# Routing digits counted with the comparisons as the stationary operand, the token list made a digit sooner, output products respread, and other orders at the seam between two experts layers

## The reference

```python
# 1. block-local attention, B=4, H=8, S=768, D=64: chunks of 32 queries see 16 left, 8 right, and 8 memory keys
# 2. mixture of experts 1: x [3072, 512], E=8, F=1024, cap = 3072 // 8 = 384
logits = x @ w_gate
order = np.argsort(-logits.flatten())
for idx in order:                                  # greedy, best logit first
    tok, e = (int(idx) // E, int(idx) % E)
    if assigned[tok] >= 0 or counts[e] >= cap:
        continue
    assigned[tok] = e
    counts[e] += 1
for e in range(E):
    out[assigned == e] = np.maximum(x[assigned == e] @ w1[e], 0.0) @ w2[e]
# 3. mixture of experts 2: noisy top-2 gating on the output of layer 2, no cap
noisy = logits + np.log1p(np.exp(x @ w_noise)) * noise
# softmax over the two best; out[token] += weight * (relu(x @ w1[e]) @ w2[e]) for each of its two experts
```

## Time and profile before

| | |
|---|---|
| time, 3 runs | 1354.14 us median (1353.6 to 1357.26) |
| profiled execution | 1354.46 us, of it 1352.7 us in the span of the profile |
| granted TensorE clock, mean | 0.959 |
| busy | PE 1241.1 us (92%), DVE 928.7 (69%), ACT 572.6 (42%), POOL 293.1 (22%) |
| attention, then the gate of layer 2 | 0 to 203 us of the span |
| routing steps n=0 and n=1 | 203 to 238, 238 to 289 us |
| routing steps n=2 to 6 | 289 to 559 us |
| `step_seventh`, `step_eighth`, `last_step` | 559 to 679 us |
| early tiles 0 and 1 of layer 3 | 679 to 730 us |
| other tiles | 730 to 1347 us, of which PE is busy 597.25 of the last 601 us |

### The profile page before, as it was taken

The page is one execution under the profiler, slowest core; times in us unless marked ns, Lnnn a source line. Parts: engine busy times, 40 slices in busy tenths (PEclk is TensorE's granted clock), DMA queues, the critical chain, the costliest instruction groups (busy, mean ns, idle before and its releaser), DMA issues.

```text
span 1352.7 us, 27991 instructions
## 1 busy us (share of the span) xinstructions
PE 1241.1 (92%) x9694; PEld 1101.9 (81%) x9694; DVE 928.7 (69%) x1924; ACT 572.6 (42%) x1232; POOL 293.1 (22%) x338
## 2 busy tenths in 40 slices
PE   7999982289999998989998999999999999999997
PEld 6888871277787876878897999898999999998986
DVE  4777756788877878754787666666666666666662
ACT  4666650133333322424323445444545455444541
POOL 3000000201102022030104324242423233232421
PEclk9999995589999999999999999999999999999999
DMA  8888853432432342444314315124252513334210
GB/s 141 165 165 164 167 129 141 141 110 80 139 111 78 132 130 72 140 150 139 87 37 157 109 55 180 40 84 144 72 175 65 196 54 116 112 103 153 80 42 18
DMA packets 174299, 154.66 MB, mean 114 GB/s; under 512 B 105117, under 2 KB 137885, under 8 KB 174240
## 3 DMA queue, kind: packets, MB, share of 16 engines
q1 hardware_dynamic: 151552, 102.83, 27.9%
q0 software_dynamic: 16128, 44.56, 10.8%
q10 hardware_dynamic: 6560, 6.49, 1.4%
HBM read 206.13 MB, written 33.75 MB: 177 GB/s over the span
## 4 chain that ended last, share of the span: by engine, by line
issue 37%; PE 33%; DVE 12%; POOL 10%; DMA 5%; ACT 2%; POOLq 1%; DVEq 0%; ACTq 0%
PE bank L784 7%; PE bank L764 6%; POOL partial L419 3%; DMA out<-result,token_now 3%; PE bank L640 3%; POOL out L423 3%; PE bank L649 2%; PE bank L628 2%; POOL held L399 2%; PE bank L710 2%; PE bank L664 2%; DMA xg<-x_dram,token_of 2%; POOL x L403 2%; PE bank L657 1%; PE bank L728 1%
## 5 line engine op out<-in xcount | busy, mean ns | idle before, releaser
L567 DVE TENSOR_TENSOR w_part<-w_sb,w_part 128x1024 fp32r<-128x1024 f32 x280 | 341.6, 1223 | 106.9 <-ACT w_part L561 99.2
L561 ACT CAST w_part<-w_sb 128x1024 fp32r<-128x1024 f32 x280 | 290.2, 1046 | 208.6 <-PE bank L1020 153.1
L995 PE MATMUL bank<-x2T,w_part 128*128 128x256 f32 x2688 | 329.3, 284 | 6.9 <-DVE h2T L1565 5.7
L995 PEld LDWEIGHTS bank<-x2T,w_part 128*128 128x128 f32 x2688 | 327.8, 193 | 9.7 <-DVE h2T L1565 5.9
L1020 PE MATMUL bank<-w_part,h2T 128*128 128x512 f32 x1344 | 312.5, 391 | 0.0
L1020 PEld LDWEIGHTS bank<-w_part,h2T 128*128 128x128 f32 x1344 | 250.2, 188 | 50.8
L784 PE MATMUL bank<-w_part,hT 128*128 128x512 f32 x576 | 157.2, 411 | 6.6 <-DVE w_part L567 5.4
L764 PE MATMUL bank<-xgT,w_part 128*128 128x384 f32 x768 | 147.3, 346 | 1.4 <-DVE hT L1219 1.1
L377 POOL DMA_INDIRECT xg<-x_dram,token_of x24 | 30.7, 1279 | 531.6 <-DVE token_of L1250 283.4
L1913 ACT ACTIVATE h2T<-bank 128x512 fp32r<-128x512 f32 x112 | 66.9, 597 | 180.6 <-PE bank L995 180.6
L764 PEld LDWEIGHTS bank<-xgT,w_part 128*128 128x128 f32 x768 | 136.0, 193 | 3.7 <-DVE hT L1219 1.6
(11 more groups left out here) (283 smaller groups left out, 1334.7 us busy)
## 6 DMA issues: line engine op xcount, KB each, us to landing
w_sb<-in_moe_w SPq DMA_DIRECT2D x280, 512.0 KB
k_in<-in_k SPq DMA_DIRECT2D x32, 240.0 KB
v_in<-in_v SPq DMA_DIRECT2D x32, 240.0 KB
q_in<-in_q SPq DMA_DIRECT2D x32, 192.0 KB
x_dram<-x_sb SPq DMA_DIRECT2D x32, 192.0 KB, 3.3
out<-zeros SPq DMA_DIRECT2D x1, 6144.0 KB, 19.7
y_dram<-y_sb ACTq DMA_DIRECT2D x24, 256.0 KB, 2.1
x<-y_dram,slot_now POOLq DMA_INDIRECT x56
```

The costliest lines, as they stand in the source:

```text
L561: scalar.copy(split_part(0, c), raw_part(c)).then_inc(hi_ready[c], 1)
L567: nc.vector.tensor_tensor(split_part(1, c), raw_part(c), split_part(0, c).bitcast(F32), ALU.subtract).then_inc(lo_ready[c], 1)
L995: last = nc.tensor.matmul(bank[2 + g % 2][:, at:at + TILE], w1_part[a][:, kt, f * P:(f + 1) * P], x2T[b][:, kt, :], start=(f % 2 == 0 and ...
```

## The change

What changes, part by part:

- **Count and vote.** In `count`, `above` (32 columns) becomes the stationary operand and `proposal` (8 columns) the moving one, so that the counts stand as 32x8 in place of 8x32. `met` is then one comparison with `room`, whose 128 partitions all hold the same row, and `room_col` goes, with PE's product for it and DVE's copy. `vote` multiplies `met` with a constant `digit_unit` [32 bins, 128] that holds the value of a bin in the digit (0 for bin 0), so its result is the digit for each expert; DVE takes the maximum of 8, for all digits but the first straight into `delta`.
- **PE's step.** The 24 output products are spread in other portions over the 14 places before and after the votes; the last two hidden tiles of j stand before and after the vote of digit 0; `sum_tokens` comes after the vote of digit 2 rather than after the count of digit 3; `turn_y` and `gate_y` move; the ranks come after one hidden tile rather than two; two hidden tiles rather than one are behind the ranks of the taken tokens.
- **DVE's step.** `taken_tiles` moves from digit 1 to digit 0, `taken_rows` from digit 2 to digits 1 and 2 before the wait for the counts, `taken_tokens` from behind `met` of digit 3 to ahead of that wait; low parts move around it.
- **Seventh, eighth, last step.** Orders on PE, DVE and ACT, as the diff shows. `gate_y(E-1, 2)` moves into tile 0.
- **GpSimd.** The fetch of tile 2's rows moves from the end of tile 0 into tile 1, behind its partial gathers.

```diff
@@ GpSimd, constants
+            for s, shift in enumerate(SHIFTS):
+                nc.gpsimd.memset(digit_unit[:, s, :], 1.0 if s == 0 else float(1 << shift)).then_inc(iota_up, 1)
             pool.wait_ge(iota_up, IOTA_OPS)
+            nc.gpsimd.memset(digit_unit[0:1, :, :], 0.0).then_inc(iota_up, 1)
@@ GpSimd, tile(j)
+                if isinstance(j, int) and j == 1:
+                    for t in range(TPE):
+                        pool.wait_ge(y_stored[t], 16 * E)
+                    pool.wait_ge(record_in, 32)
+                    pool.wait_ge(slots_ready, 2)
+                    fetch(1 - par, N)
                 for half in range(2):
                     hold(o_done, 2 * j + half + 1, 3 * j + half + 1)
...
-                if more:
-                    if isinstance(j, int) and j == 0:
-                        for t in range(TPE):
-                            pool.wait_ge(y_stored[t], 16 * E)
-                        pool.wait_ge(record_in, 32)
-                        pool.wait_ge(slots_ready, 2)
-
+                if more and not (isinstance(j, int) and j == 0):
                     fetch(par, N)
@@ PE, count, vote and step
-                    last = nc.tensor.matmul(counts[:, 0:bins], proposal[:, c, :], above[:, c, 0:bins], start=(c == 0), stop=(c == COLS - 1))
+                    last = nc.tensor.matmul(counts[0:bins, :], above[:, c, 0:bins], proposal[:, c, :], start=(c == 0), stop=(c == COLS - 1))
...
-                nc.tensor.matmul(votes_ps[:, 0:bins], ones[0:E, :], met[:, 0:bins], start=True, stop=True).then_inc(votes_up, 1)
+                nc.tensor.matmul(votes_ps, digit_unit[0:bins, s, :], met[0:bins, :], start=True, stop=True).then_inc(votes_up, 1)
...
-                before_votes = (0, 6, 10, 15, 19, 21, 23)
-                after_votes = (4, 8, 14, 18, 20, 22, 24)
+                before_votes = (0, 6, 9, 12, 15, 18, 22)
+                after_votes = (3, 8, 11, 14, 17, 20, 24)
...
                 if k is not None:
-                    for f in range(2):
-                        hidden(k, f)
+                    hidden(k, 0)
                 pe.wait_ge(tied_up, n + 1)
...
+                if k is not None:
+                    hidden(k, 1)
@@ PE, last_step
                 combine(j, 20, 24)
+                turn_x2(0, 0, 0)
                 turn_y(j, 2)
-                turn_x2(0, 0, 0)
-                gate_y(j, 2, j)
@@ DVE, step
-                    V.tensor_scalar(met[:, 0:bins], counts[:, 0:bins], room_col[:, 0:1], 1.0 if s == 0 else float(1 << shift),
-                                    ALU.is_ge, ALU.mult).then_inc(met_up, 1)
+                    V.tensor_tensor(met[0:bins, :], counts[0:bins, :], room[0:bins, :], ALU.is_ge).then_inc(met_up, 1)
...
-                    link(V.tensor_scalar(votes[:, 1:bins], votes_ps[:, 1:bins], 1.0 if s == 0 else float(1 << shift), 0.0,
-                                         ALU.min, ALU.add, accum_out=digit_f[:]))
-                    link(V.tensor_copy(delta[:], digit_f[:]))
-                    if s == 0:
+                    if s:
+                        link(V.tensor_reduce(delta[:], votes_ps, AX.X, ALU.max))
+                    else:
+                        link(V.tensor_reduce(digit_f[:], votes_ps, AX.X, ALU.max))
+                        link(V.tensor_copy(delta[:], digit_f[:]))
@@ DVE, step_seventh
                 taken_tiles(k + 1)
+                taken_rows(k + 1, 0)
                 s1_low(k, 0)
                 w_low(k, CH, 1)
+                taken_rows(k + 1, 1)
                 s1_low(k, 1)
                 w_low(k, CH + 1, 1)
                 s1_low(k, 2)
-                taken_rows(k + 1, 0)
-                taken_rows(k + 1, 1)
@@ DVE, step_eighth
+                s1_low(j, 7)
                 w_low(k, 0, 1)
-                s1_low(j, 7)
@@ ACT, last expert
+            x_high(0)
             copy_y(E - 1, 2)
             copy_yT(E - 1, 2)
-            x_high(0)
```

155 lines of the change are left out of this document (77 added, 78 removed).

## The result

The changed kernel takes 1322.71 us (median of 4, 1321.38 to 1324.13) where the kernel before takes 1355.7 (median of 4, 1353.6 to 1360.86): a ratio of 0.9743, interval 0.9706 to 0.9781. The profiled execution has a span of 1320.4 us for 1352.7.

What follows compares the result with a forecast made beforehand. PE was taken to bound the middle steps, with its waiting left to win, and the digits' chain step 1. Work and waits 14.8 plus clock 7.1 made 21.9 us off, forecast 1332.5 us, range 1326 to 1342.

Steps and rivals of the forecast that it cites:

- Step 0: Digits with nothing beside them: 0.29 us less a digit from the new vote and met, 1.9 us in all.
- Seventh and eighth step: Waits for row_hot and hT go, transpositions spread between products: 4.1 us, plus 1.5 for the low clock at 602.
- the seam: Tile 1's partial gathers, issued ahead of tile 2's fetch, let DVE run sooner: 4.7 us, plus 1.6 of clock.
- The falls of the clock in steps 4 to 6: Three falls go as stretches without wide products shrink, 1.3 us each: 3.9 us, from below 0.
- A: Rival: the clock doesn't recover or the gather stays late, gain 10 to 15 us, 1339 to 1345; chance 0.16.
- B: Rival: the count gets dearer with 32 stationary columns, so the kernel is slower, 1366 if it doubled; chance 0.02.
- C: Rival: no change, the seam's wait moves and the gains in the steps fail too; chance 0.03.
- 0.55 a step, 2.8 us for five: Steps 2 to 6: PE's waits fall from 4.0 us a step to 3.1 to 3.2; 1.2 a step at best.
- 0.5 us are left: Step 1: wide products start some 1.7 us sooner, waits at hidden tiles leave 0.5; 0.8 more for an earlier clock rise.
- 0 in sum: Last step to tile 0: the 0.95 us wait for w_part goes, waits for ACT grow; between -1.5 and 1.
- I take 0.7 off: Tile 0: transpositions and waits without wide products may bring a fall of the clock, a loss of 0.7 us.
- Each count 0.8: PE's 49 counts with above stationary and 8 moving columns: 0.8 us gained, from 0 up to 3.

Runs made afterwards that it cites:

- e9: Changed kernel with one swap in DVE's digit 1, low chunk CH+3 ahead of the low part of hidden tile 7: 1329.09 us.
- e3: Kernel before with only the new count, met and vote and no room_col, all orders as before: 1360.22 us, ratio to before 1.0028.
- e6: Changed kernel with the output products in the old portions before and after the votes: 1337.19 us.
- e7: Changed kernel with the token list made a digit later, as before: 1347.2 us.
- e15: Kernel before with only the even portions of output products, other orders and count as before: 1361.21 us, ratio to before 1.0048.
- e2: Changed kernel with PE's, DVE's and ACT's orders of the seventh, eighth and last step as before: 1332.24 us.
- e17: e9 with three useless wide products between the third count and its vote in steps 2 to 6: 1326.2 us.
- e12: Changed kernel with tile 3's fetch between tile 1's scatters, gate_y(j, 1) moved to the wait for the ties, and e9's swap: 1321.65 us.
- e13: e9 with output-product portions shifted so that one more stands between the third count and the token sums: 1322.78 us.
- e11: Changed kernel with gate_y(j, 1) moved behind hidden(k, 0), where PE waits for the ties, and ACT's copies with it: 1319.5 us.
- e4: Changed kernel with the old count, met, vote and room_col, all new orders kept: 1332.47 us.
- e14: Changed kernel with e11's gate_y move and tile 3's fetch between tile 1's scatters, without the chunk swap: 1318.67 us.
- e16: e12 with e13's portions: 1316.12 us, ratio to before 0.9719.

## Why the prediction was right and wrong

**Right.** Step 0 (2.0 for 1.9; the digit 0.34 instead of 0.29 shorter). Seventh and eighth step (5.4 for 5.6): `row_hot` and `hT` aren't waited for, and `w_part` isn't late there. The scatter and gather order of the seam: the last partial gather goes out at 690.32, the fetch behind it at 694.91, and PE's wait for `h2T` is 0.52 (forecast 1). The falls of the clock in steps 4 to 6, at 601 and at 739 are gone, all five: 3.9 + 1.5 + 1.6 were counted for them. Rivals A, B and C are out. Part of that is luck: A's argument, that the falls hang on fine things, is borne out by the neighbours of the changed kernel: e9, two swapped instructions away, has falls again. That the stretches without wide products were the cause, as the prediction had it, is not shown.

**Wrong, step by step.** The profiled span fell by 32.3 us and not 21.9. Of the 10.4 between, 5.4 are in steps 2 to 6, 3.2 in step 1, 2.0 in the last step and 1.4 ahead of step 0; the seam and the rest give some 1.4 back. The time fell out of the range because its lower end had room only for the counts and for 1.2 us a step, none for step 1 and the tail.

*"0.55 a step, 2.8 us for five ... Bounds: ... 1.2 a step at best."* Step 3 has the clock at 1.00 in both kernels and went from 53.23 to 51.50: 1.73. The mis-sized terms: `above` was laid out at 0.8 a step and is 0.6, `met` at 0.3 and isn't there, the ties at 0.9 and are 0.8 (2.5 us of waits, not 3.1 to 3.2). And the switches between sorts of products, for which 0.35 to 0.4 was given back, don't cost: PE's busy time in step 3 is 48.86, before it was 49.10.

```profile
341.51:394.74 53.23, 49.10 (x447) 41.02 (x446) 44.26 (x132) 17.28 (x29) 7.55 (x6) 1.00 0.35 114
```

Step 2 gained 1.0 only; steps 2 to 6 together make the 5.4 named above. The upper bound was the real fault: a laid-out order that is off by 0.6 us in waits can't bound a step to 1.2.

*"0.5 us are left" in step 1, and 0.8 for the clock.* It gained 4.5. The wide products start 3.4 us sooner in the step (269.01 - 234.43 = 34.58, before 275.90 - 237.88 = 38.02), not 1.7. Half of that was laid out; of the other half 1.3 are the issue of the gathers, which I took at its old length. GpSimd before and after, and the subtractions on DVE at that time in the kernel before:

```profile
258.80 1.63 POOL L377 DMA_INDIRECT xg<-x_dram,token_of  x1 [243.32 <-issue]
260.74 2.11 POOL L377 DMA_INDIRECT xg<-x_dram,token_of  x1 [0.30 <-issue]
263.15 1.54 POOL L377 DMA_INDIRECT xg<-x_dram,token_of  x1 [0.30 <-issue]
```

```profile
253.36 1.21 POOL L379 DMA_INDIRECT xg<-x_dram,token_of  x1 [235.96 <-issue]
254.88 1.55 POOL L379 DMA_INDIRECT xg<-x_dram,token_of  x1 [0.30 <-issue]
256.73 1.02 POOL L379 DMA_INDIRECT xg<-x_dram,token_of  x1 [0.30 <-issue]
```

```profile
259.46 1.23 DVE L567 TENSOR_TENSOR w_part<-w_sb,w_part 128x1024 fp32r<-128x1024 f32 x1
260.76 1.20 DVE L567 TENSOR_TENSOR w_part<-w_sb,w_part 128x1024 fp32r<-128x1024 f32 x1
263.93 1.22 DVE L567 TENSOR_TENSOR w_part<-w_sb,w_part 128x1024 fp32r<-128x1024 f32 x1
```

Before, each of the three issues has a low chunk on DVE beside it for 0.76 us or more and takes 1.54 to 2.11; after, only the second has (the chunk at 255.66) and the third takes 1.02. From list to first transposition it is 8.05 us for 9.33 (252.31 to 260.36, before 257.74 to 267.07). That DVE's chunks lengthen the issue wasn't tried by itself. Over all 48 issues of such a gather in the two traces it holds mostly: of the 24 with a chunk beside them for 0.3 us or more, 20 took 1.21 to 2.11 us; of the other 24, 23 took 0.99 to 1.03. But four with a chunk took 1.00 to 1.01, two of them (before, at 315.25 and 316.55) with 0.92 us of one, so a chunk alone doesn't decide it.

The step's tail was expected to give 1.2 back in waits; it is 1.0 shorter (12.08 for 13.10), since the clock is up sooner behind the first wide products: the first 12 take 4.19 us and the next 36 only 6.60; before, the first 24 took 7.01, by these durations some 15 of them slow.

*"0 in sum" from the last step to tile 0.* It gained 2.0, of which 0.8 is `gate_y` that has only moved into tile 0; 1.2 is left. PE's waits there are 0.24 (`x`) and 1.31 (`y_sb`) after, 0.82 (`y_sb`) and 0.73 (`x2T`) before: the same 1.55, so nothing was added against the 0.95 gained for `w_part`. After:

```profile
648.49 1.09 PE L957 MATMUL bank<-ident,x 128*128 128x128 f32 x8 [0.24 <-DMA x<-y_dram,slot_now]
650.89 0.63 PE L740 MATMUL bank<-ident,y_sb 128*128 128x128 f32 x4 [1.31 <-ACT y_sb L1768]
```

*"I take 0.7 off"* for a fall of the clock in tile 0: there is none; the granted clock is 1.00 through the transpositions and waits:

```profile
645.00:655.00 10.00, 8.45 (x60) 7.37 (x60) 2.08 (x8) 2.83 (x8) 4.96 (x6) 1.00 0.56 162
```

The Trainium skill, "TensorE: Matmul & The Clock Gate", section "Part 4: PE-mode transpose", says that transposes don't count as a busy TensorE in the same way as products; by that a fall was the likelier here. This run has 12 transpositions and 1.55 us of waits between wide products and shows none.

*The seam.* It gained 4.5 for 5.6. PE's wait for `h2T` shrank by 5.15 (4.7 was counted) and the 48 products behind it by 1.52 (1.6 counted). Against that stand the 0.8 of `gate_y` and a wait that the prediction doesn't have, 1.35 us for `x` of tile 3, whose fetch stands behind a scatter that DVE releases:

```profile
709.97 6.02 PE L1000 MATMUL bank<-x2T,w_part 128*128 128x256 f32 x48 [0.52 <-DVE h2T L1563]
717.34 1.09 PE L957 MATMUL bank<-ident,x 128*128 128x128 f32 x8 [1.35 <-DMA x<-y_dram,slot_now]
```

"What is late next" was asked of DVE alone, not of GpSimd's next fetch.

*Each count 0.8.* It gained nothing (0.69 for 0.68).

*Ahead of step 0.* The 1.4 us there can't be put down to the change: over all profiles here step 0 starts anywhere from 200.95 to 203.32.

**The sum of parts.** The prediction added terms. The runs show that they don't add: the count alone is slower by 0.3% (4 us), the even portions alone by 0.5% (6 us), count and list together faster by 1.0% (14 us); taken out of the changed kernel count, portions and list cost 9.8, 14.5 and 24.5 us. My reading: each removes the cover or the slack of another, and a step that loses it pays a second time in clock; the falls in e3, e6, e7 and e15 fit that.

What stays open: why a fall comes in one step and not in the next of equal order (before, e2 and e9 show it), whether the filler of e17 is worth anything, and the share of chance in the single differences above, since e12's fastest and slowest run (1317.68 and 1329.74) differ in their mean clock, 0.968 and 0.957.

## What to carry to other kernels

Shortening a chain pays only if what runs on its own time beside it, here a gather, is moved with it: lay out the transfer's issue and use in the new, shorter time before counting the gain. On PE, count low-clock time by windows in every run, before explaining a difference by waits: an edit that moved half a microsecond of waiting a step to another place lost 6 us in the median (e9), and other portions of the same products won them back (e13). Fill a wait with work from a place that has slack (e11), rather than shorten it by taking cover from elsewhere, and time such a kernel more than once: e12's four runs, equal in order, are 12 us apart.

## What the runs showed of the hardware

- The falls of the clock whose rows are shown here set in where small products and waits have few wide ones between them, but the same instruction order falls in one step and not in another (e9: steps 2, 4 and 6, not 3 and 5). Low time between step 2 and the seam: 20.5 us before, 0.0 after, 51.2 in e3, 37.6 in e15, 30.7 in e7, 0.0 in e4, e13, e14, e16 and e17.
- A stationary operand of 32 bf16 columns is no dearer in a series of 24 products than one of 8 (0.69 and 0.68 us), and 8 moving columns are no cheaper than 32.
- A reduction of 8 columns from PSUM into a uint32 column takes 0.17 us on DVE, as one from SBUF does.
- The issue of an indirect gather on GpSimd took 0.99 to 1.03 us in 23 of 24 cases with less than 0.3 us of a chunk's subtraction on DVE beside it, and 1.21 to 2.11 in 20 of 24 with more.
